# Products of the identity in TensorE's early waits, and value products per head, in a kernel for attention and two MLPs

## The chip, the core and the metric

One core of a Trainium2 chip runs the whole program. It has five engines that run beside each other and wait for each other by semaphores: TensorE (PE: matrix products into PSUM; its weight loads are listed as PEld), VectorE (DVE), ScalarE (ACT), GpSimd (POOL) and SyncE (SP), whose queue issues all DMAs here. The metric is the device time of one execution in microseconds; lower is better.

## The reference

Two batches, eight heads, 768 positions, head size 64. Every query sees the keys less than 16 positions away and, beside them, 24 block summaries (maximum of the keys, mean of the values over 32 positions). Two MLPs follow, 512 to 2048 to 512, with a leaky activation in the first and a rational function in the second.

```python
k_sum = k.reshape(B, H, nb, block, D).max(axis=3)
v_sum = v.reshape(B, H, nb, block, D).mean(axis=3)
scores_l = scale * q @ k.T ; mask_l = abs(pos_i - pos_j) < window
scores_s = scale * q @ k_sum.T + log(block)
a = softmax(concat(where(mask_l, scores_l, -1e9), scores_s))
x = a @ concat(v, v_sum)            # then tokens x (heads * head size)
h = x @ w_in ; g = max(h, 0) + alpha * min(h, 0) ; x = g @ w_out
h = x @ w_in2
g = (a0 + a1*h + a2*h*h + a3*h**3) / (1 + |b0|*|h| + |b1|*h*h + 1e-6)
out = g @ w_out2
```

## The kernel before

The tokens are cut into four chunks of 384 (half a batch each), the heads into four pairs: 16 jobs, job j being chunk j // 4 and pair j % 4. A job has six units of 64 queries. A unit works with 120 columns: a window of 96 keys and the 24 summaries. The stages of a job are KQ and KX (TensorE transposes keys and queries), SC (scores: one product a unit for both heads at once, since `qt` holds the queries of the two heads in opposite quarters and zeros elsewhere), NM (softmax on VectorE and ScalarE), TR (transposed probabilities, copied by ScalarE to `pt`) and PV (values).

In PV, six products a job take `vw` (120 rows, the values of both heads in 128 columns) as weights and `pt` (the probabilities of both heads, 128 columns) as the moving side. Of each output of 128x128 only two quarters are wanted, those in which the head of the values is that of the probabilities. Three units stand in each of two PSUM banks, `bk[0]` and `bk[1]`. ScalarE copies the wanted quarters to `x_hi` in four operations of 64x192 and VectorE writes the remainder to `x_lo` in four more. The MLPs work with three products for each fp32 product (hi*hi, lo*hi, hi*lo; lines 858 to 860), so that each of their operands exists as a high and a low part: `w_in_hi`, `w_in_lo`, `g_hi`, `g_lo` and so on. These products have the type fp32r, the attention's are plain fp32, and each of the latter, transposes apart, appears in the trace as two records of MATMUL and two weight loads.

The order of the work is written out by hand. Jobs 0 to 3 run first, their stages interleaved by the table FIRST_JOBS. Each of them has two PSUM banks of its own (`banks(j)`: `att`, `hid`, `acc[0:2]`, `acc[2:4]`). Parts of the first two hidden tiles of the MLP are put behind job 2's and job 3's values (EARLY). Then the loop over 64 steps of the first MLP (4 chunks, 16 tiles of 128 hidden columns) runs, and in every four steps the stages of one job of the next chunk stand between its products (SLOTS, and SOON for job 4). All jobs from 4 on use the banks `att`. The second MLP follows without attention. All loads go through SP's one queue in a written order: first keys and queries, then values, then the weights of the first MLP, the constants `alpha` and `ab`, keys of job 5, and so on. The values' last 24 rows are the block means that GpSimd makes (`vsum`), which a DMA spreads over the units.

Names: `k_raw`, `q_raw`, `kx_raw` are loaded keys and queries, `kt` and `qt` their transposes, `hid` the hidden tile's bank, `acc` those of the outputs.

Of the kernel before, what the change touches and what calls it, by code (L numbers as in the profile page):

```python
# [13 lines left out]
def attention_two_mlps(nc, q, k, v, w_in1, w_out1, alpha, w_in2, w_out2, a_coef, b_coef, out):  # L14
# [12 lines left out]
    P = 128  # L27
# [44 lines left out]
    FIRST_WEIGHTS = [(1, PV), (3, SC), (3, PV)]  # L72


    EARLY = {(2, PV): [(0, (0, 1))], (3, PV): [(0, (2,)), (1, (0, 1))]}
# [73 lines left out]
    with ExitStack() as ctx:  # L149
# [311 lines left out]
        def _(act):  # L461
# [3 lines left out]
            def attention(j, stage):  # L465
# [32 lines left out]
                elif stage == TR:  # L498
                    for g in range(2):
                        act.wait_ge(pe_t, 2 * j + g + 1)  # L500
                        if j:
                            act.wait_ge(pe_v, 2 * (j - 1) + g + 1)
                        copy(pt[0:KU, g * GU:(g + 1) * GU, :].rearrange("p u c -> p (u c)"), bk[g][0:KU, 0:GU * P]).then_inc(act_pt, 1)
                elif stage == PV:
                    for g in range(2):
                        act.wait_ge(pe_v, 2 * j + g + 1)
                        if c >= 2:
                            act.wait_ge(pe_h, (c - 1) * FT)
                        for h in range(2):
                            rows = slice(h * QT, (h + 1) * QT)  # L510
                            last = copy(x_hi[rows, c % 2, p, g * GU * QT:(g + 1) * GU * QT].rearrange("p (u r) -> p u r", u=GU),
                                        bk[g][rows, 0:GU * P].rearrange("p (u r) -> p u r", u=GU)[:, :, rows])
                        last.then_inc(act_x, 1)

# [122 lines left out]
        def _(dve):  # L637
            def attention(j, stage):
# [47 lines left out]
                elif stage == PV:  # L686
                    for g in range(2):
                        dve.wait_ge(act_x, 2 * j + g + 1)
                        for h in range(2):
                            rows, xs = slice(h * QT, (h + 1) * QT), slice(g * GU * QT, (g + 1) * GU * QT)  # L690
                            last = dve.tensor_tensor(x_lo[rows, chunk(j) % 2, p, xs].rearrange("p (u r) -> p u r", u=GU),
                                                     bk[g][rows, 0:GU * P].rearrange("p (u r) -> p u r", u=GU)[:, :, rows],
                                                     x_hi[rows, chunk(j) % 2, p, xs].bitcast(F32).rearrange("p (u r) -> p u r", u=GU),
                                                     ALU.subtract)
                        last.then_inc(dve_x, 1)

# [87 lines left out]
        def _(pe):  # L784
            def attention(j, stage):
# [4 lines left out]
                def transposes(dst, raw, raw0, rows, tiles):  # L790
# [4 lines left out]
                    return tr  # L795

                before = j - 1 if j > NPAIR else 0
                if stage == KQ:
                    if j == 0:
                        pe.wait_ge(pool_ready, 1)  # L800
                    if first:
                        pe.wait_ge(k0_loaded[p], 32)
                    else:
                        pe.wait_ge(dve_x, 2 * before + 1)
                        pe.wait_ge(k_loaded, 32 * (j - NPAIR + 1))
                    transposes(bk[0], k_raw, k_raw0, n, 4).then_inc(pe_k, 1)
                    if first:
                        pe.wait_ge(q0_loaded[p], 32)
                    else:
                        pe.wait_ge(dve_x, 2 * before + 2)  # L810
                        pe.wait_ge(q_loaded, 32 * (j - NPAIR + 1))
                    transposes(bk[1], q_raw, q_raw0, P, QTILES).then_inc(pe_q, 1)
                elif stage == KX and half(j) == 0:
                    pe.wait_ge(dve_kmax, kx_jobs(j))
                    if first:
# [19 lines left out]
                elif stage == PV:  # L835
                    if first:
                        pe.wait_ge(edges0_loaded, 32)
                        pe.wait_ge(v0_loaded[p], 32)
                        pe.wait_ge(sums0_loaded[p // 2], 16 * 4)
                    else:  # L840
                        pe.wait_ge(v_loaded[s], 96 * ((j - NPAIR) // 2 + 1))
                    for g in range(2):
                        pe.wait_ge(act_pt, 2 * j + g + 1)
                        for u in range(g * GU, (g + 1) * GU):

                            values = vw0[0:KU, u, heads(p), :] if first else vw[0:KU, s, u, :, :]
                            last = pe.matmul(bk[g][:, (u - g * GU) * P:(u - g * GU + 1) * P],  # L847
                                             values.rearrange("p h d -> p (h d)"), pt[0:KU, u, :],
                                             start=True, stop=True)
                        last.then_inc(pe_v, 1)  # L850
# [19 lines left out]
            def hidden1(i, pairs=range(KD)):  # L870
                c, f = i // FT, i % FT
                if pairs[-1] < KD - 1:

                    pe.wait_ge(dve_x, 2 * max(pairs[-1] + 1, 2))
                elif f == 0:
                    pe.wait_ge(dve_x, 2 * NPAIR * (c + 1))
                if c == 0:
# [24 lines left out]
            def hidden2(i):  # L902
# [8 lines left out]
                if i < 2:  # L911
                    pe.wait_ge(dve_x, 2 * JOBS)
                elif i < 4:
# [76 lines left out]
```

## Time and profile before

| | us |
|---|---|
| median of 3 runs | 640.69 (640.65 to 644.03) |
| the profiled execution | 642.14 |
| its span | 640.3 |
| TensorE busy in it | 616.4 (96%) |
| VectorE, ScalarE, GpSimd busy | 429.9, 330.1, 197.3 |

The span runs from the first to the last instruction; the profiled execution's own time has 1.8 us around it and lies 1.45 us above the median. A busy TensorE need not be at its peak: its records of MATMUL overlap and their ends are modelled, so what a stage costs is read from start to start, or from the chain.

### The profile page before, as it was taken

The numbers are of one execution on the slowest core, as the hardware profiler recorded it, in microseconds if no ns is written. First come the engines' busy times: TensorE is split into PE (matmuls) and PEld (weight loads), VectorE is DVE, ScalarE is ACT, GpSimd is POOL, SyncE is SP. The second block draws the span as 40 slices with busy tenths as digits, with TensorE's granted clock in tenths as the row PEclk, the third lists the DMA queues.
The fourth block names the chain that finished last, engine by engine and source line by source line (L and its number), as shares of the span: only waits on it lengthen the run. The fifth ranks groups of instructions, "written<-read, shape, count | busy, mean of one in ns | idle before, by whom it ended". The sixth has DMA issues, their size and how long they took to land.

```text
span 640.3 us, 9900 instructions
## 1 busy us (share of the span) xinstructions
PE 616.4 (96%) x3504; PEld 585.6 (91%) x3504; DVE 429.9 (67%) x992; ACT 330.1 (52%) x838; POOL 197.3 (31%) x217
## 2 busy tenths in 40 slices
PE   5778999999999999999999999999999999999998
PEld 4768899999999999999999989999999999999996
DVE  3756555656565546565555589877887788887775
ACT  4677544343333433333233287666655676557654
POOL 4544993000000000000132357443344433444331
PEclk9989999999999999999999999999999999999999
DMA  8879951122112220201244410000000010001001
GB/s 169 193 150 271 274 104 24 36 61 62 35 27 49 48 46 6 49 1 31 70 132 132 131 34 1 1 1 34 16 2 0 2 50 1 1 1 50 2 0 50
DMA packets 82209, 37.55 MB, mean 59 GB/s; under 512 B 59760, under 2 KB 76144, under 8 KB 81776
## 3 DMA queue, kind: packets, MB, share of 16 engines
q1 hardware_dynamic: 82160, 36.92, 23.3%
q8 instruction: 28, 0.46, 0.3%
q14 instruction: 21, 0.17, 0.1%
HBM read 32.58 MB, written 3.15 MB: 56 GB/s over the span
## 4 chain that ended last, share of the span: by engine, by line
PE 88%; SPq 9%; DVE 1%; DMA 1%; issue 1%; ACT 0%
PE acc L860 14%; PE acc L858 14%; PE acc L859 14%; PE hid L858 10%; PE hid L860 10%; PE hid L859 10%; PE att L858 4%; PE att L860 4%; PE att L859 3%; SPq L255 3%; PE att L847 2%; PE att L826 2%; PE att L794 1%; PE att L833 1%; SPq L304 1%; DMA q_raw<-in_q_dram 1%
## 5 line engine op out<-in xcount | busy, mean ns | idle before, releaser
L858 PE MATMUL hid<-x_hi,w_in_hi 128*128 128x384 f32 x384 | 130.5, 340 | 2.5 <-DVE g_lo L707 1.8
L859 PE MATMUL hid<-x_lo,w_in_hi 128*128 128x384 f32 x384 | 129.2, 336 | 0.0
L860 PE MATMUL hid<-x_hi,w_in_lo 128*128 128x384 f32 x384 | 129.1, 336 | 0.0
L435 POOL TENSOR_TENSOR w_out_lo<-w_out_raw,w_out_hi 128x512 fp32r<-128x512 f32 x32 | 41.2, 1289 | 247.0 <-ACT w_out_hi L463 246.7
L858 PE MATMUL acc<-g_hi,w_out_hi 128*128 128x384 f32 x256 | 90.6, 354 | 0.0
L453 POOL TENSOR_SCALAR qpart<-habs,ab 128x384 f32<-128x384 f32 x64 | 43.9, 686 | 143.1 <-ACT poly L608 142.5
L860 PE MATMUL acc<-g_hi,w_out_lo 128*128 128x384 f32 x256 | 86.7, 339 | 0.0
L859 PE MATMUL acc<-g_lo,w_out_hi 128*128 128x384 f32 x256 | 86.5, 338 | 0.0
L463 ACT ACTIVATE g_hi<-hid 128x384 fp32r<-128x384 f32 x96 | 48.3, 503 | 62.1 <-PE acc L860 54.5
L707 DVE TENSOR_TENSOR g_lo<-hid,g_hi 128x384 fp32r<-128x384 f32 x64 | 35.5, 555 | 65.8 <-ACT g_hi L463 65.8
L858 PEld LDWEIGHTS hid<-x_hi,w_in_hi 128*128 128x128 f32 x384 | 72.2, 188 | 4.4 <-issue 2.1
L860 PE MATMUL acc<-w_out_hi,g_lo 128*128 128x512 f32 x192 | 76.1, 396 | 0.0
L859 PE MATMUL acc<-w_out_lo,g_hi 128*128 128x512 f32 x192 | 75.6, 394 | 0.0
L858 PE MATMUL acc<-w_out_hi,g_hi 128*128 128x512 f32 x192 | 75.5, 393 | 0.0
L859 PEld LDWEIGHTS hid<-x_lo,w_in_hi 128*128 128x128 f32 x384 | 72.3, 188 | 1.3
L860 PEld LDWEIGHTS hid<-x_hi,w_in_lo 128*128 128x128 f32 x384 | 72.2, 188 | 0.0
L730 DVE TENSOR_SCALAR g_neg<-hid,prelu_alpha 128x384 f32<-128x384 f32 x64 | 39.4, 615 | 48.3 <-PE hid L860 46.5
L455 POOL TENSOR_TENSOR qpart<-qpart,habs 128x384 f32<-128x384 f32 x64 | 65.7, 1026 | 5.3
L859 PEld LDWEIGHTS acc<-g_lo,w_out_hi 128*128 128x128 f32 x256 | 48.2, 188 | 0.0
L858 PEld LDWEIGHTS acc<-g_hi,w_out_hi 128*128 128x128 f32 x256 | 48.2, 188 | 0.0
L860 PEld LDWEIGHTS acc<-g_hi,w_out_lo 128*128 128x128 f32 x256 | 48.1, 188 | 0.0
L495 ACT ACTIVATE att<-att,nmax 128x120 f32<-128x120 f32 x78 | 24.6, 365 | 44.4 <-DVE nmax L672 44.3
(132 smaller groups left out, 1218.5 us busy)
## 6 DMA issues: line engine op xcount, KB each, us to landing
w_in_raw<-in_moe_w_in_dram SPq DMA_DIRECT2D x32, 256.0 KB, 4.3
w_out_raw<-in_moe_w_out_dram SPq DMA_DIRECT2D x16, 512.0 KB, 4.2
vw<-in_v_dram SPq DMA_DIRECT2D x32, 120.0 KB, 3.2
q_raw<-in_q_dram SPq DMA_DIRECT2D x32, 96.0 KB, 2.9
vs_raw<-in_v_dram SPq DMA_DIRECT2D x4, 768.0 KB, 7.2
out_dram<-out_sb SPq DMA_DIRECT2D x12, 256.0 KB, 2.0
k_raw<-in_k_dram SPq DMA_DIRECT2D x16, 104.0 KB
k_raw<-in_k_dram SPq DMA_DIRECT2D x16, 100.0 KB
```

The costliest lines, as they stand in the source:

```text
L255: sp.dma_start(dst[0:rows, :, h, :], src[h].rearrange("(t p) d -> p t d", p=rows)).then_inc(loaded, 16)
L435: pool.tensor_tensor(w_out_lo[:, f, :], w_out_raw[:, f, :], w_out_hi[f][:, :].bitcast(F32), ALU.subtract).then_inc(pool_w_out, 1)
L453: pool.tensor_scalar(qpart[:, i % 2, :], habs[:, i % 2, :], ab[:, 5:6], ab[:, 4:5], ALU.mult, ALU.add).then_inc(pool_qb, 1)
L455: pool.tensor_tensor(qpart[:, i % 2, :], qpart[:, i % 2, :], habs[:, i % 2, :], ALU.mult).then_inc(pool_q, 1)
L463: return act.activation(dst, src, ACT.Identity)
L495: last = act.activation(scores_of(bk, g, u), scores_of(bk, g, u), ACT.Exp, scale=-1.0, bias=nmax[:, s, u:u + 1], accum_out=sums_of(bk, g)[ ...
L707: dve.tensor_tensor(g1_lo[:, i % R1, :], hid[i % 2][:, 0:CH], g1_hi[:, i % R1, :].bitcast(F32), ALU.subtract).then_inc(dve_g, 1)
L730: dve.tensor_scalar(g_neg[:, :], hb, 0.0, prelu_alpha[:, f:f + 1], ALU.min, ALU.mult).then_inc(dve_m, 1)
L826: last = pe.matmul(bk[g][:, (u - g * GU) * KU:(u - g * GU + 1) * KU], qt[:, s, u, :], kt[:, s, u, :], start=True, stop=True)
L858: pe.matmul(dst, lhs[0], rhs[0], start=start, stop=False)
L859: pe.matmul(dst, lhs[0], rhs[1], start=False, stop=False)
L860: return pe.matmul(dst, lhs[1], rhs[0], start=False, stop=stop)
```

## The change

It has two parts.

Run-up products. A table RUN_UP says for six places among the first jobs how many products of the identity with itself (128x128, fp32) TensorE makes there. Their results go to a bank that nothing else uses at that time (`acc[3]` in the stages KQ and KX, `bk[1]` in PV), and nobody reads them. They stand ahead of the waits for that stage's data. In PV of the first four jobs a wait until both halves of `pt` are copied is put ahead of them.

Value products per head. Each of the six products of a job becomes two, one a head: 64 weight columns, 64 moving columns, and an output of 64 rows and 64 columns, in the upper or the lower half of the rows of `bk[0]`. All six units fit into one bank, `bk[0]`; `bk[1]` isn't written. ScalarE and VectorE copy it in one operation of 128x384 each, once all products are done, and the semaphores `act_x` and `dve_x` count jobs instead of halves of jobs. The transposes of the queries in KQ, which go to `bk[1]`, wait for ScalarE's copy of the job before's `pt` instead of VectorE's `x_lo`.

```diff
--- before.py
+++ after.py
@@ -71,6 +71,8 @@
 
     FIRST_WEIGHTS = [(1, PV), (3, SC), (3, PV)]
 
+
+    RUN_UP = {(0, KQ): 6, (0, KX): 2, (1, KX): 1, (2, KQ): 4, (0, PV): 6, (2, PV): 8}
 
     EARLY = {(2, PV): [(0, (0, 1))], (3, PV): [(0, (2,)), (1, (0, 1))]}
 
@@ -502,15 +504,10 @@
                             act.wait_ge(pe_v, 2 * (j - 1) + g + 1)
                         copy(pt[0:KU, g * GU:(g + 1) * GU, :].rearrange("p u c -> p (u c)"), bk[g][0:KU, 0:GU * P]).then_inc(act_pt, 1)
                 elif stage == PV:
-                    for g in range(2):
-                        act.wait_ge(pe_v, 2 * j + g + 1)
-                        if c >= 2:
-                            act.wait_ge(pe_h, (c - 1) * FT)
-                        for h in range(2):
-                            rows = slice(h * QT, (h + 1) * QT)
-                            last = copy(x_hi[rows, c % 2, p, g * GU * QT:(g + 1) * GU * QT].rearrange("p (u r) -> p u r", u=GU),
-                                        bk[g][rows, 0:GU * P].rearrange("p (u r) -> p u r", u=GU)[:, :, rows])
-                        last.then_inc(act_x, 1)
+                    act.wait_ge(pe_v, 2 * (j + 1))
+                    if c >= 2:
+                        act.wait_ge(pe_h, (c - 1) * FT)
+                    copy(x_hi[:, c % 2, p, :], bk[0][:, 0:CH]).then_inc(act_x, 1)
 
             def slot(c, f, n):
 
@@ -684,15 +681,9 @@
                         dve.tensor_tensor(probs[:, s, us, :], bk[g][:, 0:GU * KU].rearrange("p (u k) -> p u k", u=GU),
                                           prec[:, s, us].unsqueeze(2).broadcast_to([P, GU, KU]), ALU.mult).then_inc(dve_p, 1)
                 elif stage == PV:
-                    for g in range(2):
-                        dve.wait_ge(act_x, 2 * j + g + 1)
-                        for h in range(2):
-                            rows, xs = slice(h * QT, (h + 1) * QT), slice(g * GU * QT, (g + 1) * GU * QT)
-                            last = dve.tensor_tensor(x_lo[rows, chunk(j) % 2, p, xs].rearrange("p (u r) -> p u r", u=GU),
-                                                     bk[g][rows, 0:GU * P].rearrange("p (u r) -> p u r", u=GU)[:, :, rows],
-                                                     x_hi[rows, chunk(j) % 2, p, xs].bitcast(F32).rearrange("p (u r) -> p u r", u=GU),
-                                                     ALU.subtract)
-                        last.then_inc(dve_x, 1)
+                    dve.wait_ge(act_x, j + 1)
+                    dve.tensor_tensor(x_lo[:, chunk(j) % 2, p, :], bk[0][:, 0:CH], x_hi[:, chunk(j) % 2, p, :].bitcast(F32),
+                                      ALU.subtract).then_inc(dve_x, 1)
 
             def slot(c, f, n):
                 for j, stage in stages(c, f, n):
@@ -794,23 +785,30 @@
                         tr = pe.transpose(dst[:, t * rows:(t + 1) * rows], rows_of_pair.rearrange("p h d -> p (h d)"), ident[0:rows, 0:rows])
                     return tr
 
+                def run_up(dst):
+
+                    for _ in range(RUN_UP.get((j, stage), 0)):
+                        pe.matmul(dst[:, 0:P], ident[:, :], ident[:, :], start=True, stop=True)
+
                 before = j - 1 if j > NPAIR else 0
                 if stage == KQ:
                     if j == 0:
                         pe.wait_ge(pool_ready, 1)
+                    run_up(acc[3])
                     if first:
                         pe.wait_ge(k0_loaded[p], 32)
                     else:
-                        pe.wait_ge(dve_x, 2 * before + 1)
+                        pe.wait_ge(dve_x, before + 1)
                         pe.wait_ge(k_loaded, 32 * (j - NPAIR + 1))
                     transposes(bk[0], k_raw, k_raw0, n, 4).then_inc(pe_k, 1)
                     if first:
                         pe.wait_ge(q0_loaded[p], 32)
                     else:
-                        pe.wait_ge(dve_x, 2 * before + 2)
+                        pe.wait_ge(act_pt, 2 * before + 2)
                         pe.wait_ge(q_loaded, 32 * (j - NPAIR + 1))
                     transposes(bk[1], q_raw, q_raw0, P, QTILES).then_inc(pe_q, 1)
                 elif stage == KX and half(j) == 0:
+                    run_up(acc[3])
                     pe.wait_ge(dve_kmax, kx_jobs(j))
                     if first:
                         pe.wait_ge(kx0_loaded[p], 32)
@@ -834,6 +832,8 @@
                         last.then_inc(pe_t, 1)
                 elif stage == PV:
                     if first:
+                        pe.wait_ge(act_pt, 2 * (j + 1))
+                        run_up(bk[1])
                         pe.wait_ge(edges0_loaded, 32)
                         pe.wait_ge(v0_loaded[p], 32)
                         pe.wait_ge(sums0_loaded[p // 2], 16 * 4)
@@ -842,11 +842,10 @@
                     for g in range(2):
                         pe.wait_ge(act_pt, 2 * j + g + 1)
                         for u in range(g * GU, (g + 1) * GU):
-
-                            values = vw0[0:KU, u, heads(p), :] if first else vw[0:KU, s, u, :, :]
-                            last = pe.matmul(bk[g][:, (u - g * GU) * P:(u - g * GU + 1) * P],
-                                             values.rearrange("p h d -> p (h d)"), pt[0:KU, u, :],
-                                             start=True, stop=True)
+                            for h in range(2):
+                                rows = slice(h * QT, (h + 1) * QT)
+                                values = vw0[0:KU, u, 2 * p + h, :] if first else vw[0:KU, s, u, h, :]
+                                last = pe.matmul(bk[0][rows, u * QT:(u + 1) * QT], values, pt[0:KU, u, rows], start=True, stop=True)
                         last.then_inc(pe_v, 1)
 
             def slot(c, f, n):
@@ -871,9 +870,9 @@
                 c, f = i // FT, i % FT
                 if pairs[-1] < KD - 1:
 
-                    pe.wait_ge(dve_x, 2 * max(pairs[-1] + 1, 2))
+                    pe.wait_ge(dve_x, max(pairs[-1] + 1, 2))
                 elif f == 0:
-                    pe.wait_ge(dve_x, 2 * NPAIR * (c + 1))
+                    pe.wait_ge(dve_x, NPAIR * (c + 1))
                 if c == 0:
                     pe.wait_ge(pool_w_in, f + 1)
                 if i >= 2:
@@ -909,7 +908,7 @@
                 if n == 0:
                     pe.wait_ge(dve_w_in, f + 1)
                 if i < 2:
-                    pe.wait_ge(dve_x, 2 * JOBS)
+                    pe.wait_ge(dve_x, JOBS)
                 elif i < 4:
                     pe.wait_ge(dve_g, STEPS - 4 + i + 1)
                 else:
```

TensorE at the values of job 0 (`att0` and `att1` are its banks, `vw0` its values), before:

```order
L847 MATMUL att0<-pt_108,vw0_49 128x128 [waits sums0_loaded0,act_pt,v0_loaded0,edges0_loaded]
L847 MATMUL att0<-pt_108,vw0_49 128x128 x2
L847 MATMUL att1<-pt_108,vw0_49 128x128 [waits act_pt]
L847 MATMUL att1<-pt_108,vw0_49 128x128 x2
L847 MATMUL hid0<-pt_108,vw0_49 128x128 [waits sums0_loaded0,act_pt,v0_loaded1,edges0_loaded]
L847 MATMUL hid0<-pt_108,vw0_49 128x128 x2
L847 MATMUL hid1<-pt_108,vw0_49 128x128 [waits act_pt]
L847 MATMUL hid1<-pt_108,vw0_49 128x128 x2
```

and now:

```order
L791 MATMUL att1<-ident_97 128x128 [waits act_pt]
L791 MATMUL att1<-ident_97 128x128 x5
L848 MATMUL att0<-pt_108,vw0_49 64x64 [waits sums0_loaded0,act_pt,v0_loaded0,edges0_loaded]
L848 MATMUL att0<-pt_108,vw0_49 64x64 x5
L848 MATMUL att0<-pt_108,vw0_49 64x64 [waits act_pt]
L848 MATMUL att0<-pt_108,vw0_49 64x64 x5
L848 MATMUL hid0<-pt_108,vw0_49 64x64 [waits sums0_loaded0,v0_loaded1,act_pt,edges0_loaded]
L848 MATMUL hid0<-pt_108,vw0_49 64x64 x5
L848 MATMUL hid0<-pt_108,vw0_49 64x64 [waits act_pt]
L848 MATMUL hid0<-pt_108,vw0_49 64x64 x5
```

Six products of the identity and their wait for `act_pt` came ahead, the six products of 128 columns became twelve of 64 in one bank.

TensorE from the scores of job 3 (`acc2`, `acc3`) over the values of job 2 (`acc0`, `acc1`) to the first hidden tile, before:

```order
L826 MATMUL acc2<-kt_102,qt_103 128x120 [waits dve_ks,act_q,act_k]
L826 MATMUL acc2<-kt_102,qt_103 128x120 x2
L826 MATMUL acc3<-kt_102,qt_103 128x120 x3
L847 MATMUL acc0<-pt_108,vw0_49 128x128 [waits sums0_loaded1,act_pt,v0_loaded2,edges0_loaded]
L847 MATMUL acc0<-pt_108,vw0_49 128x128 x2
L847 MATMUL acc1<-pt_108,vw0_49 128x128 [waits act_pt]
L847 MATMUL acc1<-pt_108,vw0_49 128x128 x2
L858 MATMUL hid0<-x_hi_90,w_in_hi0_51 128x384 [waits pool_w_in,dve_x]
```

and now:

```order
L824 MATMUL acc2<-kt_102,qt_103 128x120 [waits dve_ks,act_q,act_k]
L824 MATMUL acc2<-kt_102,qt_103 128x120 x2
L824 MATMUL acc3<-kt_102,qt_103 128x120 x3
L791 MATMUL acc1<-ident_97 128x128 [waits act_pt]
L791 MATMUL acc1<-ident_97 128x128 x7
L848 MATMUL acc0<-pt_108,vw0_49 64x64 [waits sums0_loaded1,act_pt,v0_loaded2,edges0_loaded]
L848 MATMUL acc0<-pt_108,vw0_49 64x64 x5
L848 MATMUL acc0<-pt_108,vw0_49 64x64 [waits act_pt]
L848 MATMUL acc0<-pt_108,vw0_49 64x64 x5
L857 MATMUL hid0<-x_hi_90,w_in_hi0_51 128x384 [waits pool_w_in,dve_x]
```

Eight products of the identity stand between the scores and the values, behind a wait for `act_pt` and ahead of the waits for the loads `sums0_loaded1` and `v0_loaded2`.

ScalarE in the same place, from the weights to job 3's output, before:

```order
L463 ACTIVATE w_out_hi1_73<-w_out_raw_88 128x512
L463 ACTIVATE x_hi_90<-acc0 64x192 x2
L463 ACTIVATE x_hi_90<-acc1 64x192 x2
L463 ACTIVATE pt_108<-acc2 120x384
L463 ACTIVATE pt_108<-acc3 120x384
L463 ACTIVATE kt_102<-att0 128x5x96
L463 ACTIVATE kt_102<-att0 128x80
L463 ACTIVATE qt_103<-att1 64x6x64 x2
L463 ACTIVATE x_hi_90<-acc2 64x192 x2
L463 ACTIVATE x_hi_90<-acc3 64x192 x2
L463 ACTIVATE w_in_hi2_53<-w_in_raw_67 128x512
L463 ACTIVATE w_out_hi2_74<-w_out_raw_88 128x512
```

and now:

```order
L465 ACTIVATE w_out_hi1_73<-w_out_raw_88 128x512
L465 ACTIVATE x_hi_90<-acc0 128x384
L465 ACTIVATE pt_108<-acc2 120x384
L465 ACTIVATE pt_108<-acc3 120x384
L465 ACTIVATE kt_102<-att0 128x5x96
L465 ACTIVATE kt_102<-att0 128x80
L465 ACTIVATE qt_103<-att1 64x6x64 x2
L465 ACTIVATE x_hi_90<-acc2 128x384
L465 ACTIVATE w_in_hi2_53<-w_in_raw_67 128x512
L465 ACTIVATE w_out_hi2_74<-w_out_raw_88 128x512
```

Each job's output is one copy instead of four; the rest stands as it stood.

## Rows read from the trace of the kernel before

**Rows 1.** The page: busy time by engine, share of the span, instructions.
```profile
PE 616.4 (96%) x3504; PEld 585.6 (91%) x3504; DVE 429.9 (67%) x992; ACT 330.1 (52%) x838; POOL 197.3 (31%) x217
```

**Rows 2.** Busy time (x instructions) in three stretches; us, engines, granted clock, DMA share, GB/s.
```profile
0.00:66.00 66.00, 46.78 (x289) 42.78 (x289) 38.43 (x138) 41.38 (x135) 33.12 (x42) 0.97 0.89 197
66.00:335.00 269.00, 268.84 (x1692) 267.97 (x1693) 152.76 (x427) 106.83 (x333) 40.83 (x38) 1.00 0.25 61
335.00:640.30 305.30, 300.79 (x1525) 274.87 (x1523) 238.70 (x428) 181.85 (x371) 123.33 (x139) 1.00 0.08 27
```

**Rows 3.** The chain that ended last, in order of time: start us, us, what.
```profile
71.94 1.33 PE att L826 x12
...
81.29 1.34 PE att L847 x12
...
98.36 0.65 PE att L833 x6
...
131.44 0.30 PE att L794 x4
...
291.50 1.34 PE att L847 x12
```

**Rows 4.** TensorE in order: start us, us, line, operation, out<-in; idle before and its releaser.
```profile
3.98 0.93 PE L794 MATMUL att<-ident,k_raw 104*128 104x104 f32 x4 [3.98 <-DMA k_raw<-in_k_dram]
...
11.14 2.82 PE L826 MATMUL att<-kt,qt 128*128 128x120 f32 x12
...
27.74 1.58 PE L847 MATMUL att<-pt,vw 120*128 120x128 f32 x12 [1.72 <-DMA vw<-in_v_dram]
...
36.77 2.90 PE L847 MATMUL acc<-pt,vw 120*128 120x128 f32 x12 [3.82 <-DMA vw<-vsum]
...
45.88 0.45 PE L858 MATMUL hid<-x_hi,w_in_hi 128*128 128x384 f32 x1 [0.69 <-DVE x_lo L691]
...
50.91 0.41 PE L858 MATMUL hid<-x_hi,w_in_hi 128*128 128x384 f32 x1 [1.83 <-DVE g_lo L707]
...
65.35 0.54 PE L794 MATMUL att<-ident,k_raw 100*128 100x100 f32 x4 [1.67 <-DMA k_raw<-in_k_dram]
66.16 0.52 PE L794 MATMUL att<-ident,q_raw 128*128 128x128 f32 x3 [0.27 <-DMA q_raw<-in_q_dram]
```

**Rows 5.** VectorE in order of time, the same columns.
```profile
44.35 1.48 DVE L691 TENSOR_TENSOR x_lo<-acc,x_hi 64x192 fp32r<-64x192 f32 x4 [2.96 <-ACT x_hi L463]
47.69 0.62 DVE L730 TENSOR_SCALAR g_neg<-hid,prelu_alpha 128x384 f32<-128x384 f32 x1 [1.86 <-DMA ab<-in_moe_b_dram]
...
50.22 0.55 DVE L707 TENSOR_TENSOR g_lo<-hid,g_hi 128x384 fp32r<-128x384 f32 x1
```

**Rows 6.** The DMA queue's own issues in order of time.
```profile
38.78 4.87 SPq L358 DMA_DIRECT2D ab<-in_moe_a_dram  x1
43.69 0.44 SPq L359 DMA_DIRECT2D ab<-in_moe_b_dram  x1
```

**Rows 7.** ScalarE in order of time, around the third value job and the fourth.
```profile
34.88 0.87 ACT L463 ACTIVATE pt<-acc 120x384 f32<-120x384 f32 x2
...
43.65 1.35 ACT L463 ACTIVATE x_hi<-acc 64x192 fp32r<-64x192 f32 x4
```

**Rows 8.** TensorE's busy time and granted clock around 36 us; columns as in rows 2.
```profile
35.00:36.00 1.00, 0.00 (x0) 1.00 1.09 160
...
37.00:38.00 1.00, 1.00 (x6) 0.50 0.98 204
...
40.00:41.00 1.00, 1.00 (x7) 0.97 0.93 238
```

**Rows 9.** TensorE in order around one value stage.
```profile
80.95 0.34 PE L860 MATMUL hid<-x_hi,w_in_lo 128*128 128x384 f32 x1
81.12 1.50 PE L847 MATMUL att<-pt,vw 120*128 120x128 f32 x12
82.38 0.42 PE L858 MATMUL acc<-g_hi,w_out_hi 128*128 128x384 f32 x1
```

## The prediction

> **What bounds the kernel now.** The page first: TensorE is busy for 616.4 of 640.3 us and no other engine for more than 430 [rows 1]. A share over the whole run hides that it has two parts, so the second view is the busy time by stretch [rows 2]. In the first 66 us TensorE works 46.78 us, while the DMA engines are at a share of 0.89. From 66 to 335 us, where jobs 5 to 15 run between the products of the first MLP, it is busy 268.84 of 269.00 us at the full granted clock (2.4 GHz). Behind that comes no attention at all. What shortens TensorE's own work after 66 us shortens the run; what shortens ScalarE or VectorE there meets an engine that never waits for them.
>
> Third the chain of waits [rows 3]: the value products of a job are 12 records in 1.34 us, and eleven jobs (5 to 15, first row at 81.29, last at 291.50) have them in the chain. All of that is TensorE.
>
> Then the first 66 us in order of time, TensorE's waits with their releasers [rows 4]. The six places of the run-up are among them. What matters more is which waits end at a time that TensorE doesn't set:
> - 27.74, job 0's values: a DMA.
> - 36.77, job 2's values: the DMA of the block means, after 3.82 us of idling.
> - 50.91, the third hidden tile: it waits for g_lo, and VectorE's row explains why. VectorE began its first MLP work at 47.69, released by the DMA of the coefficients `ab` [rows 5], whose issues had occupied the queue from 38.78 to 44.13 [rows 6]. From 47.69 VectorE's own order (two MLP operations, six score operations, g_lo at 50.22) leads to 50.91.
> - 65.35 and 66.16, keys and queries of job 5: DMAs, after 1.67 and 0.27 us of idling [rows 4].
>
> **The run-up products and the earlier releases: nothing at the end.** Each run-up product is 128 columns of fp32 in two records. At full clock two records cost 2 x 1.34/12 = 0.22 us [rows 3]; at half clock 0.43, since twelve score records took 2.82 us at 11.14 (2.82/6 = 0.47, with the last one's tail) [rows 4]. There are 27: 6, 2, 1, 4, 6 and 8.
> - The six ahead of job 0's keys start when the identity is made and take 2.6 to 2.8 us at half clock, about what the 3.98 us wait leaves. They and the seven behind them may bring the clock up earlier than now, and the score products of jobs 0 and 1 could drop from 2.8 to about 1.5 us. All of it ends at 27.74, which a DMA sets.
> - The six ahead of job 0's values cost 1.3 us in a wait of 1.72.
> - The eight ahead of job 2's values wait for ScalarE's copies of its transposes, which end at 34.88 + 0.87 = 35.75 [rows 7], and take 1.8 us: until 37.5, 0.8 past the load at 36.77. In return the clock should not fall. Now it does: granted 1.00 at 35 us, 0.50 (1.2 GHz) from 37 to 40, back at 40 [rows 8], and the values took 2.90 us instead of 1.50. TensorE gains 1.4 - 0.8 and some 0.3 on the next products, about 0.9 us by 41 us.
> - Job 3's output: ScalarE's four pieces (1.35 us at 43.65 [rows 7]) become one, VectorE's four (1.48 us at 44.35 [rows 5]) become one. A 128x384 g_lo takes 0.55 us, so VectorE saves 0.9 and ScalarE about as much. The wait at 45.88 goes and TensorE is about 1.7 us ahead.
> - At 50.91 it is all taken back. TensorE stops near 47.4 instead of 49.1 and idles 3.5 us instead of 1.83 until VectorE, released by a DMA, has g_lo. What would still pass through meets the wait at 65.35. No load up to there waits for anything that TensorE does late, so the DMAs land when they land now.
> - One added wait: the value products of jobs 0 to 3 now begin when both halves of `pt` are copied, not the first; 0.4 us at most, half of ScalarE's 0.87 [rows 7], and behind it stand only products that end before 65.35.
> I cost the whole beginning at 0. If that cover were gone, the most it could give is the idle time at 65.35 and 66.16, 1.9 us. The other end: an idle time of 3.5 us is close to the 3.8 after which the clock fell. If it falls at 50.9, three and a half us at half clock lose 1.7 us, and the 1.94 us at 65.35 and 66.16 cover that too. So 0, between -1.9 and +1.7.
>
> **The value products per head: the term that counts.** Before, 6 products a job of 128 weight columns and 128 moving columns, of which half the output is thrown away. Now 12 products of 64 and 64, alternating between the upper and the lower half of the output rows: 24 records instead of 12, each with half the columns. No row shows a record of 64 columns, so I bound it.
> - Does a record's cost follow its columns? Transposes of 128 columns cost 0.65/6 = 109 ns each, those of 88 columns 0.30/4 = 76 ns [rows 3]: 0.70 of the time for 0.69 of the columns, with no floor yet. Continued to 64 that is 55 ns, and 24 x 0.055 = 1.33 us, the same as now.
> - Upper end: a record of 64 costs as much as one of 88. 24 x 0.076 = 1.82, +0.48 us a job.
> - Lower end: products for the two halves of the rows run side by side: 0.67 us, -0.67 a job. Against it: score records have 120 moving columns and value records 128, yet twelve take 1.33 and 1.34 us [rows 3]. The pace there isn't the moving side's alone; the weight loads (128 columns in both) set it too. To halve the time both must run side by side.
> - The edges. The first MLP product after a value stage lasts 0.42 us, the one ahead of the stage 0.34 [rows 9]: a change of kind costs about 0.08. The new shape makes entry and exit one step bigger; I take 0.08 at each, 0.16 a job.
> The nearest rows are the transposes, so I take 0 for the products and 0.16 for the edges: 11 x 0.16 = +1.8 us. Jobs 0 to 4 run before the wait at 65.35 and count nothing. ScalarE's and VectorE's saved 0.8 to 0.9 us a job lie beside a busy TensorE and bring nothing.
>
> **Sum.** The profiled execution took 642.14 us (span 640.3 and 1.8 around it); 0 + 1.8 gives 643.9. It was 1.45 us above the median of the runs, 640.69, so for the median I say 642.5.
>
> **Rivals.**
> 1. Slower: the array has to empty before it works in halves and again after. What now overlaps is lost at each change. The row shows how much: the value stage's last record ends at 81.12 + 1.50 = 82.62, 0.24 us after the next product began at 82.38 [rows 9]. Lost at entry and exit, 0.48 us a job, 11 x 0.48 = 5.3: 646.0. With the floor of 88 columns as well it would be 651.3. It decides from 0.29 us a job on. For it: the shape changes twice in every job, between products that follow without a gap. Against it: the change of type shown costs only 0.08.
> The Trainium skill, TensorEngine Tiling, Key Properties, says that changing the tiling mode drains TensorE. No row here shows such a change; by that rule the time is this rival's, 646.
> 2. Faster: both halves side by side, -0.67 + 0.16 a job, 11 x -0.51 = -5.6: 635.1, or 633.3 without edges. For it: neighbouring products write different halves of the rows. Against it: the weight loads, as above, and two records of each product share a half.
> The same section of the Trainium skill says that different tiles can load weights and multiply in parallel. No row shows it; it would give this rival's 633 to 635.
> 3. The beginning does count: the wait at 65.35 shrinks or moves, up to -1.9 us: 638.8. Against it: the DMA share of 0.89 and the DMA named as releaser.
>
> **How the numbers follow.** Half a per cent, 3.2 us, is what a measurement can tell from no change: 637.5 and 643.9 are the marks. Forecast, 0 to +0.29 us a job, 640.7 to 643.9: 0.44. Rival 1, 643.9 to 650: 0.29. Rival 2, 633.3 to 637.5: 0.19. Rival 3 or halves partly side by side, 637.5 to 640.7: 0.08. So faster 0.19, same 0.52, slower 0.29. The range leaves out the outer part of both rivals: 635.5 to 647. The forecast's own is 640.7 to 643.9.
>
> **What would show it.** After: the value stage in the chain (1.34 us now) and the start of the product behind it; the waits at 27.74, 36.77, 50.91 and 65.35, whose ends should stand within 0.8 us while the idle time at 50.91 grows; the granted clock at 37 to 40 us, which should be full; ScalarE's and VectorE's output copies at about 0.5 us each. A value stage of 1 us or less makes the prediction wrong on the fast side, one of 1.7 or more on the slow side, and an end of the wait at 65.35 that comes more than 1 us earlier says that the beginning wasn't tied to DMAs.

## The result

| | before | changed |
|---|---|---|
| median, us | 640.77 (639.08 to 644.03, 20 runs) | 638.35 (635.75 to 641.11, 20 runs) |
| ratio | | 0.9953 (0.9939 to 0.9967) |
| profiled execution, span | 642.14, 640.3 | 637.51, 635.7 |

The change makes the kernel 0.47% faster, with 0.33 to 0.61% as the interval (2.1 to 3.9 us). The ratio is that of the averages, 638.34 and 641.34 us; the medians lie 2.42 us or 0.38% apart. 642.5 was predicted, 640.7 to 643.9 as the forecast's own range.

The busy time by stretch in the profile of the changed kernel (columns as in [rows 2]):

```profile
0.00:66.00 66.00, 49.86 (x411) 46.13 (x412) 33.47 (x123) 38.16 (x123) 34.29 (x43) 0.95 0.88 204
66.00:330.40 264.40, 264.40 (x1817) 259.98 (x1817) 141.99 (x393) 96.88 (x297) 39.91 (x37) 1.00 0.25 60
```

TensorE is busy without a gap from 66 to 330.4 us; before it was busy for 268.84 of 269.00 us there [rows 2]. The chain of waits of the changed kernel (start us, us, what), which answers to [rows 3]:

```profile
70.56 1.33 PE att L824 x12
...
79.93 0.85 PE att L848 x24
...
96.70 0.66 PE att L831 x6
...
129.21 0.30 PE att L785 x4
...
287.19 0.85 PE att L848 x24
```

A value stage has 24 records in 0.85 us where it had 12 in 1.34. Scores (1.33), probabilities (0.66) and keys (0.30) are as they were. From the first value stage to the last, ten jobs, it is 287.19 - 79.93 = 207.26 us; before it was 291.50 - 81.29 = 210.21 [rows 3]. That is 0.295 us a job.

TensorE in order around one value stage of the changed kernel (start us, us, line, what), answering to [rows 9]:

```profile
141.72 0.34 PE L859 MATMUL hid<-x_hi,w_in_lo 128*128 128x384 f32 x1
141.99 0.92 PE L848 MATMUL att<-pt,vw 120*64 120x64 f32 x24
142.83 0.44 PE L857 MATMUL acc<-g_hi,w_out_hi 128*128 128x384 f32 x1
143.11 0.34 PE L858 MATMUL acc<-g_lo,w_out_hi 128*128 128x384 f32 x1
```

The stage costs 0.84 us from its start to the next product's (before: 82.38 - 81.12 = 1.26 [rows 9]). The edges got dearer: the last hidden product ahead of it started 0.27 us ahead of it instead of 0.17, and the product behind it takes 0.28 to the next start instead of 0.26 (82.64 in the trace before).

TensorE in order of time in the first 66 us of the changed kernel, answering to [rows 4]; L791 is the products of the identity:

```profile
9.56 1.53 PE L824 MATMUL att<-kt,qt 128*128 128x120 f32 x12
...
34.78 2.05 PE L791 MATMUL acc<-ident 128*128 128x128 f32 x16 [2.91 <-ACT pt L465]
36.76 0.92 PE L848 MATMUL acc<-pt,vw 120*64 120x64 f32 x24
...
49.16 0.41 PE L857 MATMUL hid<-x_hi,w_in_hi 128*128 128x384 f32 x1 [3.19 <-DVE g_lo L698]
...
50.87 0.52 PE L859 MATMUL hid<-x_hi,w_in_lo 128*128 128x384 f32 x1
...
64.31 0.53 PE L785 MATMUL att<-ident,k_raw 100*128 100x100 f32 x4 [1.14 <-DMA k_raw<-in_k_dram]
64.78 0.52 PE L785 MATMUL att<-ident,q_raw 128*128 128x128 f32 x3
```

VectorE in the same trace, answering to [rows 5]:

```profile
45.93 0.62 DVE L721 TENSOR_SCALAR g_neg<-hid,prelu_alpha 128x384 f32<-128x384 f32 x1 [3.20 <-DMA ab<-in_moe_b_dram]
...
48.46 0.55 DVE L698 TENSOR_TENSOR g_lo<-hid,g_hi 128x384 fp32r<-128x384 f32 x1
```

and TensorE's busy time with its granted clock, answering to [rows 8]:

```profile
37.00:38.00 1.00, 1.00 (x26) 1.00 0.87 253
...
51.00:52.00 1.00, 1.00 (x5) 0.50 1.09 332
```

The first scores take 1.53 us at full clock instead of 2.82 [rows 4]. The clock is now full where it was half (37 to 40 us [rows 8]), and the values of job 2 take 0.92 us. But TensorE then idles 3.19 us for g_lo instead of 1.83, since VectorE still begins its MLP work when the DMA of `ab` lands (45.93), and behind that idle time the clock falls: 0.50 at 51, and a product of 384 columns takes 0.52 us instead of 0.34. The queries of job 5 begin at 64.78 instead of 66.16; behind them the span has 635.7 - 64.78 = 570.92 us against 640.3 - 66.16 = 574.14. So the two profiled executions differ by 3.2 us behind that point and by 1.4 ahead of it. The experiments show that the 3.2, which lie inside the interval above, belong to the change; the 1.4 lie within the spread of single executions.

### The profile page after: what moved, and what is told of

It reads as the page before. It is cut to its first block, busy times and chain, and to the rows that moved or that the text cites. A ratio compares the mean times of both kernels' runs of the same rounds, so it can differ in the third digit from the quotient of the medians.

```text
span 635.7 us, 10287 instructions
## 1 busy us (share of the span) xinstructions
PE 615.0 (97%) x3750; PEld 580.9 (91%) x3750; DVE 414.3 (65%) x944; ACT 317.4 (50%) x790; POOL 197.8 (31%) x217
## 4 chain that ended last, share of the span: by engine, by line
PE 88%; SPq 8%; DMA 1%; DVE 1%; issue 1%; ACT 0%
PE acc L857 14%; PE acc L859 14%; PE acc L858 14%; PE hid L857 10%; PE hid L859 10%; PE hid L858 10%; PE att L857 4%; PE att L859 4%; PE att L858 4%; SPq L257 3%; PE att L824 2%; PE att L848 1%; PE att L785 1%; DMA k_raw<-in_k_dram 1%; PE att L831 1%; SPq L306 1%
```

## The experiments

e1 to e4 share one set of runs of the kernel before, e5 to e7 another, e8 to e10 a third; the runs of the changed kernel above had a set of their own. Ratios are to the set's kernel before.

**e1 and e2: one part alone.** In e1 the run-up table is empty and the wait ahead of it gone:

```diff
-    RUN_UP = {(0, KQ): 6, (0, KX): 2, (1, KX): 1, (2, KQ): 4, (0, PV): 6, (2, PV): 8}
+    RUN_UP = {}
-                        pe.wait_ge(act_pt, 2 * (j + 1))
-                        run_up(bk[1])
```

> The changed kernel without its 27 products of the identity and without the wait for pt put ahead of them; the value products per head stay. Theory: what the change brings is the value stage alone, 1.69 us from start to start before and 1.40 after, 0.29 us in each of the eleven jobs behind 66 us, 3.2 us in all. Then this kernel is 3.2 us below the kernel before (637.5, ratio 0.995), a value stage in the chain has 0.85 us, and it isn't slower than the changed kernel. Rival: the run-up products bring part of the gain (the wait for job 5's keys ended 1.0 us earlier in the profile of the changed kernel). Then this kernel lies 1 us or more above the changed one, near 639.5.

Measured: 640.28 us, ratio 0.9967 (0.9946 to 0.9988). The interval holds the theory's 0.995, and the value stage in its chain has 0.85 us, but the median is nearer to the rival's 639.5 than to 637.5. In its profile the queries of job 5 begin at 63.62, with 634.5 - 63.62 = 570.88 us of span behind them, as in the changed kernel (570.92).

e2 is the kernel before with the table, the function `run_up`, its calls and the wait added, and nothing else:

```diff
+    RUN_UP = {(0, KQ): 6, (0, KX): 2, (1, KX): 1, (2, KQ): 4, (0, PV): 6, (2, PV): 8}
+                    run_up(acc[3])          # KQ and KX, ahead of their waits
+                        pe.wait_ge(act_pt, 2 * (j + 1))
+                        run_up(bk[1])
```

> The kernel before with the 27 products of the identity at the same six places and the wait for pt ahead of those in the value stages; the value products and the copies are as before. Theory: nothing at the end, 640.8 within 0.7 us, ratio 1.000: the granted clock is full at 37 to 40 us, TensorE waits longer at 50.9 and the keys of job 5 end it all. A value stage in the chain has 1.34 us. Rival, run-up gives: 639.5 or less, with the wait for job 5's keys ending earlier by 1 us or more. Rival, run-up costs: 641.5 or more.

Measured: 642.15 us, ratio 1.0008 (0.9989 to 1.0027). The run-up alone is no change. TensorE in e2, at the values of job 2 and at the keys of job 5:

```profile
35.04 2.05 PE L802 MATMUL acc<-ident 128*128 128x128 f32 x16 [2.01 <-ACT pt L465]
36.93 1.50 PE L858 MATMUL acc<-pt,vw 120*128 120x128 f32 x12
```

```profile
64.30 0.54 PE L796 MATMUL att<-ident,k_raw 100*128 100x100 f32 x4 [0.43 <-DMA k_raw<-in_k_dram]
64.87 0.52 PE L796 MATMUL att<-ident,q_raw 128*128 128x128 f32 x3
```

In this profile the products of the identity did what they are for: job 2's values took 1.50 us instead of 2.90 [rows 4]. They don't do it every time, and the clock can stay up without them. In e3, further down, which has the same products, the clock was half (0.50) from 37 to 39 us and they took 3.42 us themselves; in e10, which has none, it stayed full over the wait of 3.00 us. The first row is e3, the second e10:

```profile
35.77 3.42 PE L791 MATMUL acc<-ident 128*128 128x128 f32 x16 [2.39 <-ACT pt L465]
```

```profile
35.83 0.92 PE L846 MATMUL acc<-pt,vw 120*64 120x64 f32 x24 [3.00 <-DMA vw<-vsum]
```

The first scores took 2.82 us in e2 (at 11.15), no less than before. The queries of job 5 began at 64.87, near the changed kernel's 64.78, but the span behind them is 639.0 - 64.87 = 574.13 us, as before.

**e9 and e10: the changed kernel and e1 once more, beside the same runs of the kernel before**, since e1's interval alone didn't tell whether the run-up brings something beside the new products.

> The changed kernel itself, in the same call as the kernel with per-head products alone, so that both stand beside the same runs of the kernel before. Theory: the run-up products bring nothing that can be measured; ratio 0.995, within 0.001 of e10. Rival, they bring 0.5 us or more: 0.0015 or more below e10.

> The kernel e1 again (per-head products, no products of the identity). Theory: ratio 0.995 to 0.9965 and within 0.001 of e9. Rival: 0.0015 or more above e9.

Measured: e9 638.68 us, 0.9958 (0.9940 to 0.9977); e10 638.11 us, 0.9948 (0.9927 to 0.9968). In e9's profile the queries of job 5 began at 66.11, with 637.1 - 66.11 = 570.99 us of span behind them; in e10's at 64.50, with 635.4 - 64.50 = 570.90. Without the run-up the kernel is not slower; the difference of 0.001 lies inside both intervals. What TensorE waits for in e10 (us in total, times, longest):

```profile
PE hid L855 <- DVE g_lo L698: 3.8, 1, 3.8
...
PE acc L846 <- DMA vw<-vsum: 3.0, 1, 3.0
```

Without the run-up products the wait for the block means (3.0 us) and the wait for g_lo (3.8) are both there, and cost nothing at the end. The wait for g_lo is even longer than with them (3.19 in the changed kernel, 3.53 in e9).

**e4: per-head products with the old copies.**

```diff
-                            values = vw0[0:KU, u, heads(p), :] if first else vw[0:KU, s, u, :, :]
-                            last = pe.matmul(bk[g][:, (u - g * GU) * P:(u - g * GU + 1) * P], ...)
+                            for h in range(2):
+                                rows, c0 = slice(h * QT, (h + 1) * QT), (u - g * GU) * P + h * QT
+                                values = vw0[0:KU, u, 2 * p + h, :] if first else vw[0:KU, s, u, h, :]
+                                last = pe.matmul(bk[g][rows, c0:c0 + QT], values, pt[0:KU, u, rows], start=True, stop=True)
```

> The kernel before with two value products for each one (64 weight columns, 64 moving columns, 64 output rows, one head each), written to the places where the wanted quarters stood, in two banks; eight copies a job as before, no run-up. Theory: TensorE's stage is all of the gain: ratio 0.995, 637.5, value stage 0.85 us in the chain, jobs in the steady part 0.29 us shorter. Rival: part of the gain comes from the fewer and larger copies of ScalarE and VectorE or from the one bank; then this kernel lies 0.5 us or more above the one with per-head products and single copies (e1).

Measured: 639.29 us, 0.9957 (0.9937 to 0.9977), against 0.9967 of e1 beside the same runs. The first and last value stage in its chain:

```profile
81.08 0.85 PE att L848 x24
...
288.35 0.85 PE att L848 x24
```

The same 0.85 us, and (288.35 - 81.08) / 10 = 20.73 us a job as in the changed kernel. One bank and single copies bring nothing that can be measured at the end; the products are the gain. What the single copies do change is a wait. With the old copies TensorE still waits for `x_lo` at 44.55 (0.99 us) and then 2.16 us for g_lo; in e2, which has them too, these were 0.44 and 1.98 us. With single copies, e1 and e10, the wait for `x_lo` is gone and the one for g_lo has 3.86 and 3.85 us. The rows at g_lo in e4, e2 and e10:

```profile
49.90 0.66 PE L857 MATMUL hid<-x_hi,w_in_hi 128*128 128x384 f32 x1 [2.16 <-DVE g_lo L707]
```

```profile
49.58 0.41 PE L869 MATMUL hid<-x_hi,w_in_hi 128*128 128x384 f32 x1 [1.98 <-DVE g_lo L709]
```

```profile
48.94 0.66 PE L855 MATMUL hid<-x_hi,w_in_hi 128*128 128x384 f32 x1 [3.85 <-DVE g_lo L698]
```

**e3: the same products, one head after the other.**

```diff
+                    pe.wait_ge(act_pt, 2 * (j + 1))
+                    for h in range(2):
+                        for u in range(UNITS):
                             ...
-                    for g in range(2):
-                        pe.wait_ge(act_pt, 2 * j + g + 1)
-                        for u in range(g * GU, (g + 1) * GU):
-                            for h in range(2):
                                 ...
```

Both signals to ScalarE now come among the second head's six products.

> The changed kernel with the twelve value products of a job in another order: the six of one head (upper half of the output rows), then the six of the other, instead of taking turns. Theory, halves side by side: products work beside each other only where neighbours use different halves, so the 24 records take about 24 x 0.055 = 1.3 us instead of 0.85, and the run is 11 x 0.45 = 5 us above the changed kernel. Rival, small records are just cheaper: a record of 64 columns costs 0.035 us whatever its half, the stage stays at 0.85 us and the time is unchanged.

Measured (one run): 645.67 us. Its first and last value stage in the chain, and TensorE around one:

```profile
82.55 1.36 PE att L847 x24
...
294.88 1.36 PE att L847 x24
```

```profile
103.31 0.34 PE L859 MATMUL hid<-x_hi,w_in_lo 128*128 128x384 f32 x1
103.58 1.44 PE L847 MATMUL att<-pt,vw 120*64 120x64 f32 x24
104.94 0.44 PE L857 MATMUL acc<-g_hi,w_out_hi 128*128 128x384 f32 x1
```

24 records of the same size take 1.36 us when neighbours share a half of the array and 0.85 when they take turns. 1.36 / 24 = 57 ns, which is what the prediction had continued from the transposes (55). Per job it is (294.88 - 82.55) / 10 = 21.23 us, 0.51 above the changed kernel, 5.6 us for eleven, where the theory had 5; it is also 0.21 above the kernel before (21.02). (The rest of its distance, some 1.7 us, lies at 66 to 100 us, where its granted clock was 0.95.) The entry costs 0.27 us here too, so the edge comes from the shape of the products and not from their order.

**e5: twice the moving columns.**

```diff
+                            for h in range(2):
+                                rows, c0 = slice(h * QT, (h + 1) * QT), (u - g * GU) * P
+                                values = vw0[0:KU, u, 2 * p + h, :] if first else vw[0:KU, s, u, h, :]
+                                last = pe.matmul(bk[g][rows, c0:c0 + P], values, pt[0:KU, u, :], start=True, stop=True)
```

> The kernel before, each value product split by head in its weights alone: twelve products a job with 64 weight columns, all 128 moving columns and 64 output rows, taking turns between the halves; outputs and copies as before. It doubles the moving side of the changed kernel's records. Theory, records of opposite halves work side by side: only every second record waits for its own half, so 24 records of 128 moving columns take 12 to 13 x 0.107 = 1.3 to 1.5 us, about what twelve wide records took before, and the run stays at 640 to 643. Rival, what was saved came from cheaper small records and not from working side by side: 24 x 0.107 = 2.6 us a stage and 11 x 1.25 = 14 us more in the run.

Measured (one run): 646.79 us; the value stages in its chain:

```profile
82.70 1.46 PE att L848 x24
...
295.90 1.46 PE att L848 x24
```

24 records of 128 moving columns take 1.46 us, 61 ns each. Twelve records of 128 moving columns after one another took 1.34 [rows 3], so 24 would take 2.7. They do work beside each other, nearly two at a time. (The twelve had 128 weight columns and these have 64; what that alone is worth no run shows, and e3 against the changed kernel doesn't need it.) The stage came as the theory had it, the time over 643 didn't. A job takes (295.90 - 82.70) / 10 = 21.32 us, 0.30 more than before: 0.12 in the stage (1.46 against 1.34) and the rest at its edges, 3.3 us for eleven. Another 1.7 us are a spell of low clock (granted 0.95 from 66.5 to 100 us).

**e6, e7, e8: what does move the beginning.** The changed kernel with loads in another order. e7 puts the keys and queries of job 5 ahead of the third block of raw values; e6 moves the constants too; e8 adds to e6 that GpSimd sums the third block two weight tiles later. The queries of job 5 began between 63.62 and 66.16 in the profiles of all kernels with the old order of loads.

```diff
             load_keys(4)
+            sp.dma_start(prelu_alpha ...); sp.dma_start(ab[:, 0:4] ...); sp.dma_start(ab[:, 4:6] ...)   # e6, e8
             load_w(0, 1)
             ...
             load_w(0, 4)
+            load_keys(5)            # e6, e7, e8
             load_v_blocks(2)
-            load_keys(5)
             ...
-                if f in (5, 11):
+                if f in (7, 11):    # e8
```

> The changed kernel with only the keys and queries of job 5 moved ahead of the third block of raw values. Theory: the keys land up to 3.8 us earlier (768 KB at about 200 GB/s), TensorE doesn't wait at job 5's keys any more, 1.1 us or, in other executions, up to 2 us: ratio about 0.993. Rival: the wait turns up elsewhere, at the weights of tiles 6 and 7 behind GpSimd's sums, and the ratio stays at 0.995.

Measured: 637.19 us, 0.9930 (0.9908 to 0.9952). TensorE at the queries of job 5 and at the first wait behind them:

```profile
62.63 0.49 PE L785 MATMUL att<-ident,q_raw 128*128 128x128 f32 x3
...
72.28 0.44 PE L857 MATMUL hid<-x_hi,w_in_hi 128*128 128x384 f32 x1 [1.48 <-POOL w_in_lo L432]
```

TensorE doesn't wait for job 5's keys any more and the ratio is the theory's, but the rival's wait is there too, 1.48 us for `w_in_lo`.

> The changed kernel with two loads moved forward in the queue: the constants (alpha, a, b) ahead of the second pair of weight tiles, the keys and queries of job 5 ahead of the third block of raw values. Theory: the beginning ends where DMAs end, so only this moves it. VectorE's first MLP work begins up to 2.7 us earlier (at the end of the first hidden tile, 43.2 in the profile of the changed kernel, instead of 45.9) and the wait of 1.1 us for job 5's keys goes: 1 to 3 us below the changed kernel, ratio 0.991 to 0.994 to the kernel before. Rival, the loads as a whole bound the beginning and another one is late in their place (weights, values of job 4 or the last raw values): no gain against the changed kernel, ratio 0.995.

Measured: 637.51 us, 0.9936 (0.9912 to 0.9960). VectorE's first MLP operation, and TensorE's waits for g_lo, for job 5 and behind it:

```profile
42.99 0.62 DVE L721 TENSOR_SCALAR g_neg<-hid,prelu_alpha 128x384 f32<-128x384 f32 x1 [0.96 <-PE hid L859]
```

```profile
47.50 0.41 PE L857 MATMUL hid<-x_hi,w_in_hi 128*128 128x384 f32 x1 [2.23 <-DVE g_lo L698]
...
61.05 0.52 PE L785 MATMUL att<-ident,q_raw 128*128 128x128 f32 x3 [0.65 <-DMA q_raw<-in_q_dram]
...
70.89 0.45 PE L857 MATMUL hid<-x_hi,w_in_hi 128*128 128x384 f32 x1 [1.67 <-POOL w_in_lo L432]
```

VectorE starts at 42.99, released by TensorE and no longer by the DMA. The queries of job 5 begin at 61.05. But 1.67 us come back as a wait for `w_in_lo`, which GpSimd makes behind its sums; part theory, part rival. The ratios of e6 and e7 overlap in their intervals with the changed kernel's (0.9953; 0.9939 to 0.9967), so the times alone don't show a gain over it; the traces do, and then e8's time.

> The kernel with constants and job 5's keys loaded earlier (e6), and GpSimd's sums over the third block of raw values moved behind the weight tiles 6 and 7 instead of ahead of them. Theory: in e6 the saved wait came back as a wait of 1.7 us for w_in_lo of tile 6, behind these sums; now it goes, and the run is about 1.5 us below e6, ratio 0.990 to 0.992. Rival, SP's queue waits for the sums before it loads the fourth block and the keys of job 6, so that a wait for these takes the place: ratio 0.9935 as e6, with a wait for k_raw in the trace behind 80 us.

Measured: 635.52 us, 0.9907 (0.9884 to 0.9929), the fastest of all. What TensorE waits for behind 66.5 us:

```profile
PE att L857 <- DVE g_lo L736: 1.4, 1, 1.4
PE att L785 <- DMA q_raw<-in_q_dram: 0.8, 1, 0.8
PE att L785 <- DMA k_raw<-in_k_dram: 0.5, 1, 0.5
```

The wait for `w_in_lo` is gone; 1.3 us for the keys and queries of a later job, which stand in the queue behind the sums, are new, as the rival had it. So e8 has gained little on e6 in the traces: behind the start of job 5's queries (61.12 and 61.05) lie 572.48 us of span against 572.85. Beside the same runs the changed kernel had 0.9958 (e9), outside e8's interval: the whole is 0.9% on the kernel before, half of it from the order of the work of SP and GpSimd together.

## Why the prediction was wrong

**The products of the value stage: the step that failed.** The term was 0 for the products, with -0.67 a job as the lower end, and 0.16 for the edges. In the chain, where the prediction read its 1.34, the stage went to 0.85, -0.49. The whole job became 0.295 us shorter, which leaves about 0.2 for the edges. (From start to start the same sum reads 1.26 to 0.84 for the stage and 0.10 and 0.02 for the edges.) 11 x -0.295 = -3.2 us instead of +1.8. The sign that I had named for the fast side, a value stage of 1 us or less, is met.

The step went wrong in one inference. The cost of a record does follow its columns (57 ns measured in e3, 55 estimated). But from scores of 120 moving columns and values of 128 taking equally long, I concluded that the weight loads set the pace, and I held that against the overlap. No row showed that they can't go beside each other. That loads of 128 columns set a pace of 0.11 us a record had even a row against it: the four records of 0.30 us [rows 3] are transposes of 88 moving columns, each with a load of 128 weight columns, at about 76 ns. e3 and e5 show that records of opposite halves, their weight loads included, do go beside each other: 0.85 against 1.36 us for nothing but another order. e3 is also the kernel that the sum described, one without overlap, and it lies 0.21 us a job above the kernel before, near the sum's 0.16. So this one step carries the miss.

I named the overlap as rival 2 with 0.19 and priced it in full; the truth lay between, at -0.49 of -0.67, in the strip to which I had given 0.08. Why it isn't the full half stays open. The two records of one product share a half, and e5 with longer records comes nearer to it (1.46 of 1.34 x 2), so a cost per record would fit, but no run measured that by itself.

**The edges: right.** They cost 0.12 us from start to start, about 0.2 in the chain, against 0.16 in the sum; rival 1 asked for 0.48. The overlap that it priced did shrink, and that is in these figures: the last record ended 0.24 us after the next product's start before, 141.99 + 0.92 - 142.83 = 0.08 now. The Trainium skill, TensorEngine Tiling (Array Packing), Key Properties, says that changing the tiling mode drains TensorE; if it does, both changes together cost no more than this here, not the 0.48 of a fully lost overlap. The same section's sentence that tiles load and multiply in parallel agrees with e3 and e5, and was the one to weigh more.

**The run-up products: right in the sum, in part by other ways.** e2 puts them at 1.0008, with 0.2% to either side. The steps came out in the profile of the changed kernel: the clock is full at 37 to 40 us, and TensorE reaches the wait for g_lo earlier and idles 3.19 us (3.5 predicted). But the longer wait is the work of the single copies, which the same term held, and not of the run-up: 1.98 us in e2, 3.86 and 3.85 in e1 and e10. And whether the clock stays up is not settled by the run-up products: e3 has them and fell to half, e10 has none and didn't. Where the clock fell behind the wait for g_lo, which was the other end of the bounds, the wait for job 5 covered it in the changed kernel (1.14 us of idling left).

**One sign was drawn too narrow.** I wrote that a wait for job 5 ending over 1 us earlier would show that the beginning isn't tied to DMAs. In the changed kernel's profile it ended 1.04 us earlier, the landing of `ab` came 1.8 us earlier, and the wait at 50.91 ended at 49.16, so that the 0.8 us allowed for its end didn't hold either. But the queries of job 5 began at 66.16, 64.78 and 66.11 in the profiles of before, changed and changed again, and at 63.62 and 64.50 in e1 and e10, one kernel without any run-up. That spread is one of executions; the DMAs land at other times each time. e6 to e8 speak for a beginning that is tied to them: with moved loads the queries began at 61.05 to 62.63, earlier than in any kernel where only products had changed.

**ScalarE's and VectorE's copies: right,** nothing at the end (e4 against e1).

## What to carry to other kernels

Where only two opposite quarters of a product's output are wanted, split it into two products of half the weight columns and half the moving columns, and let neighbours take turns between the halves of the output rows; the order alone was worth 0.51 us in a stage of 1.36. Before filling a wait with work that keeps the clock up, follow the saved time to the next wait and ask what releases that one: here it was a DMA twice, and beside the split products only another order of loads, with GpSimd's sums, moved the end. An overlap that no row of a trace excludes belongs into the sum's middle and not only to its lower end.

## What was not expected of the hardware

Plain fp32 records of 64 by 64 columns over 120 rows went at 35 ns each taking turns, and at 57 ns in the same half.

And the clock can fall after a shorter idle time than 3.8 us, but the length of the idle time alone doesn't settle it. At the wait for g_lo it fell behind 1.98 us in e2 (0.50 at 51 us) and 2.16 in e4, and stayed full behind 2.33 in e7 and 2.25 in e5. And in e5 TensorE waited 2.11 us for job 5's keys, the transposes of the keys still ran at full speed and those of the queries, 0.49 to 0.52 us in the other kernels, took 0.72. From 66 to 72 us the granted clock was 0.72 on average there, and the same in e3, where two waits of 0.96 and 0.95 us stood before it; 6 x 0.28 = 1.7 us that nothing behind covers. In the profiles of before and changed it was 1.00 at that place, though before had waited 1.67 and 0.27 us there. TensorE in e5:

```profile
65.29 0.53 PE L794 MATMUL att<-ident,k_raw 100*128 100x100 f32 x4 [2.11 <-DMA k_raw<-in_k_dram]
65.99 0.72 PE L794 MATMUL att<-ident,q_raw 128*128 128x128 f32 x3 [0.17 <-DMA q_raw<-in_q_dram]
```
